# One-hot matmuls move the last chunk's rows into expert 0's slots; the kept slots are turned ahead of the ranks

## The reference

```
# 1. clustered attention: q, k, v (2, 8, 768, 64), 16 centroids per head
mask = argmax(q_n @ c_n) == argmax(k_n @ c_n)            # same nearest centroid
attn = softmax(where(mask, scale * q @ k.T, -1e9)) @ v    # -> x (1536, 512)
# 2. dense layer, w_in (512, 2048), w_out (2048, 512)
h = x @ w_in;  x = (h * sigmoid(1.702 * h)) @ w_out
# 3. mixture of 8 experts, two for each token, w1 (8, 512, 1024), w2 (8, 1024, 512)
noisy = x @ w_gate + log1p(exp(x @ w_noise)) * noise
top2 = two largest of noisy; weights = softmax of the two
out[token] = sum over its two experts of weight * (relu(x @ w1[e]) @ w2[e])
```

## Time and profile before

| | |
|---|---|
| median of 3 runs | 946.74 us (945.55 to 947.07) |
| the profiled execution's own time | 947.12 us |
| its span, first to last instruction | 945.3 us |
| mean granted TensorE clock | 0.971 of full |
| PE busy | 900.9 us, 95% of the span |
| DVE, ACT, POOL busy | 525.3, 420.4, 137.9 us |

### The profile page before, as it was taken

How to read it: one execution, slowest core, us unless ns; L and a number is a source line. 1 busy time by engine, 2 the same in 40 slices (tenths; PEclk the granted TensorE clock), 3 DMA queues, 4 the chain that set the end, 5 groups by cost and what they waited for, 6 DMA issues and landing times.

```text
span 945.3 us, 12455 instructions
## 1 busy us (share of the span) xinstructions
PE 900.9 (95%) x4314; PEld 732.3 (77%) x4315; DVE 525.3 (56%) x949; ACT 420.4 (44%) x685; POOL 137.9 (15%) x144
## 2 busy tenths in 40 slices
PE   6999999999999999999999991999999999999995
PEld 4777777777766888888888881888888888888884
DVE  7787878888755443456345533445344443444373
ACT  4667777676774332352235230424344243424320
POOL 2021221222121000005000504100000000005072
PEclk7999999999999999999999995899999999999998
DMA  5132432333174222325332534325263453428364
GB/s 121 38 92 75 124 92 52 120 90 94 41 236 165 97 89 89 134 90 178 90 133 89 179 109 150 130 90 175 85 206 114 146 178 116 166 89 285 121 220 146
DMA packets 84301, 118.98 MB, mean 126 GB/s; under 512 B 19258, under 2 KB 47930, under 8 KB 84256
## 3 DMA queue, kind: packets, MB, share of 16 engines
q1 hardware_dynamic: 79328, 104.08, 34.2%
q0 software_dynamic: 4928, 14.35, 4.4%
HBM read 89.12 MB, written 29.39 MB: 125 GB/s over the span
## 4 chain that ended last, share of the span: by engine, by line
PE 86%; DVE 8%; issue 2%; DMA 2%; ACT 1%; POOL 1%; SPq 0%; POOLq 0%; DVEq 0%; ACTq 0%
PE psum L867 10%; PE psum L868 10%; PE psum L869 10%; PE psum L881 9%; PE psum L783 9%; PE psum L882 9%; PE psum L883 9%; PE psum L748 3%; PE psum L768 3%; PE psum L769 3%; PE psum L1012 2%; DVE neg_max L1364 2%; PE psum L879 1%; PE psum L878 1%; PE psum L725 1%
## 5 line engine op out<-in xcount | busy, mean ns | idle before, releaser
L783 PE MATMUL psum<-probs,vx 128*128 128x386 f32 x384 | 155.8, 487 | 0.3 <-ACT probs L1078 0.3
L881 PE MATMUL psum<-down_hi,hid_hi 128*128 128x512 f32 x384 | 151.3, 394 | 0.0
L882 PE MATMUL psum<-down_lo,hid_hi 128*128 128x512 f32 x384 | 149.8, 390 | 0.0
L883 PE MATMUL psum<-down_hi,hid_lo 128*128 128x512 f32 x384 | 149.8, 390 | 0.0
L1243 ACT ACTIVATE hid_hi<-psum 128x448 fp32r<-128x448 f32 x64 | 34.8, 544 | 185.5 <-PE psum L869 185.5
L1078 ACT ACTIVATE probs<-psum 128x384 f32<-128x384 f32 x192 | 90.2, 488 | 54.9 <-PE psum L769 52.9
L1364 DVE TENSOR_REDUCE neg_max<-psum 128x1 f32<-128x768 f32 x96 | 91.3, 955 | 24.4 <-PE psum L748 20.7
L1646 DVE SCALAR_TENSOR_TENSOR hid_lo<-psum,hid_hi 128x384 fp32r<-128x384 f32 x64 | 35.6, 557 | 124.0 <-ACT hid_hi L1243 124.0
L1217 ACT ACTIVATE gelu<-psum 128x512 f32<-128x512 f32 x48 | 28.7, 598 | 158.9 <-PE psum L869 158.9
L867 PE MATMUL psum<-sx_hi,up_hi 128*128 128x448 f32 x256 | 94.7, 370 | 0.0
L868 PE MATMUL psum<-sx_lo,up_hi 128*128 128x448 f32 x256 | 94.5, 369 | 0.0
(11 more groups left out here) (194 smaller groups left out, 1495.1 us busy)
## 6 DMA issues: line engine op xcount, KB each, us to landing
raw<-in_moe_w SPq DMA_DIRECT2D x64, 512.0 KB, 4.3
raw<-in_moe_w_in SPq DMA_DIRECT2D x24, 512.0 KB, 3.4
raw<-in_moe_w_out SPq DMA_DIRECT2D x24, 512.0 KB, 5.1
slot_x<-zeros SPq DMA_DIRECT2D x7, 1024.0 KB, 5.5
slot_rows<-slot_x SPq DMA_DIRECT2D x8, 768.0 KB, 5.3
raw_q<-in_q SPq DMA_DIRECT2D x30, 192.0 KB, 3.4
raw_k<-in_k SPq DMA_DIRECT2D x30, 192.0 KB, 3.7
slot_y<-y_sb SPq DMA_DIRECT2D x7, 768.0 KB, 3.8
```

Of the source, the lines that this page charges most:

```text
L783: mm(psum[:, 5 + half, 0:WIDE], vx[:, n % 2, c], probs[:, at % SLOTS], start=(c == 0), stop=(c == J - 1)).then_inc(unit_done, 1)
L881: mm(dst, hid_hi[:, f % 2, cols], down_hi[:, slot, f % GP], start=(f == 0), stop=False)
L882: mm(dst, hid_hi[:, f % 2, cols], down_lo[:, slot, f % GP], start=False, stop=False)
L883: return mm(dst, hid_lo[:, f % 2, cols], down_hi[:, slot, f % GP], start=False, stop=(f == pieces - 1))
```

## The change

**Attention's end.** Of head 15's four splits, only the two of weight group 0 stand ahead of `head_result(15, 0)`; the two of group 1 come behind it.

**Expert 0's slots.** SP loads them after the last chunk's weight loads, when the low scatters of chunks 0 and 1 have landed (`slot_x` holds zeros in slots not yet taken). So `slot_rows` has the rows that the first two chunks put there. After the last chunk's `logits`, PE puts these "kept" slots in place with 16 matmuls against the identity (`kept_slots`, banks 4 to 7). They are ordinary float32 matmuls, no transposes, since the banks must go on accumulating. Then come the `ranks`. The last chunk's rows never go through DRAM for expert 0: ACT and DVE split `y_sb` into `row_hi` and `row_lo` (8 operations of 128x512, in the space of `xt_hi` and `xt_lo`); `first_moves` on DVE makes for each of the four tiles of tokens a matrix of ones and zeros (128 tokens by 448 slots) from `slot_of` and `key`; and `move_rows` on PE does 32 matmuls of 448 columns (4 blocks of features by 4 tiles by hi and lo) that add the rows to the banks. `place` comes behind `first_moves`; between its slot numbers and its weights DVE now does `turn_lo` for two of the four blocks, and for the other two at its end. The 16 transposes of expert 0's slots are gone.

**Queues.** POOL makes `slot_of` and waits for `sx_in` before it scatters the last chunk. SP's `expert_step` loads the next expert's slots behind the first two of its weight groups, not ahead of them, and first waits for all scatters.

**The end.** `hid_hi` and `hid_lo` get a third buffer for the last piece of the last expert; `down_end` takes the last three pieces tile by tile, and `ORDER` is 0, 3, 1, 2 everywhere.

```diff
--- before.py
+++ after.py
...
-        ORDER = (FULL,) + tuple(range(FULL))
+        ORDER = (0, FULL) + tuple(range(1, FULL))
...
+        def row_hi(j):
+
+            return xt_hi[:, j, 0:CT]
...
+        def moves(j):
+
+            return xt_hi[:, j, CT:CT + CAP]
...
-            keep_rows(t)
...
+            sp.wait_ge(scattered_low, (CHUNKS - 1) * (DMA * TPC))
+            load_slots(0, 0)
+            keep_rows(t)
+
             def expert_step(r, e, last):
                 n = r * E + e
                 if not last:
 
-                    when(sx_done, n * DC + DC)
-                    load_slots(r, e + 1)
                     for i in range(EGR):
+                        if i == STAGES:
+                            when(sx_done, n * DC + DC)
+                            sp.wait_ge(scattered_low, DMA * TILES)
+                            sp.wait_ge(scattered, DMA * TILES)
+                            load_slots(r, e + 1)
                         load_group(weights_of(e + 1, i), EXPERT0 + n * EGR + i + RING, i % STAGES)
...
-            sp.wait_ge(scattered_low, DMA * TILES)
-            load_slots(0, 0)
-            sp.wait_ge(scattered, DMA * TILES)
...
+
+            with pool.Fori(0, CHUNKS - 1) as t:
+                scatter_chunk(t)
+            chain.link(nc.gpsimd.iota(slot_i[:], pattern=[[1, CAP]], base=-FAR, channel_multiplier=0))
+            nc.gpsimd.tensor_copy(slot_of[:], slot_i[:]).then_inc(slot_of_set, 1)
+            pool.wait_ge(sx_in, 2 * DMA)
+            scatter_chunk(CHUNKS - 1)
...
-            def down_end(f, slot, piece, pieces):
...
+            def down_end(piece0, pieces):
+
                 for i, j in enumerate(ORDER):
-                    if i == 2:
-                        down_tile(f - 1, slot, True, ORDER[3], pieces)
-                    last = down_tile(f, slot, True, j, pieces)
-                    if i < TPC - 1:
+                    for f in range(pieces - 3, pieces):
+                        if i == 0:
+                            pe.wait_ge(hid_done, piece0 + f + 1)
+                        last = down_tile(f, f // GP % RING, True, j, pieces, 2 if f == pieces - 1 else None)
+                        if i == YT - 1 and f % GP == GP - 1:
+                            last.then_inc(group_used, 1)
+                    if i < YT - 1:
                         last.then_inc(y_ready, 1)
...
-                    if f >= 1:
+                    if f >= 1 and not (end and f == pieces - 2):
                         down(f - 1, ((f - 1) // GP) % RING, rest, piece0 + f - 1, pieces)
...
+                pe.wait_ge(sx_in, 2 * DMA)
+                for c in range(DC):
+                    kept_slots(c)
                 ranks(p, LAST)
+                for c in range(DC):
+                    move_rows(c)
+
+            def kept_slots(c):
+
+                for j in range(YT):
+                    rows = rows_of(j)
+                    mm(psum[:, turn_bank(c, True), j * P:j * P + rows], slot_rows[0:rows, j, c * P:(c + 1) * P],
+                       ident[0:rows, 0:rows], start=(j == 0), stop=False)
+
+            def move_rows(c):
+
+                dst = psum[:, turn_bank(c, True), 0:CAP]
+                for j in range(TPC):
+                    if c == 0:
+                        pe.wait_ge(split_lo, j + 1)
+                        pe.wait_ge(moves_ready, j + 1)
+                    mm(dst, row_hi(j)[:, c * P:(c + 1) * P], moves(j), start=False, stop=False)
+                    last = mm(dst, row_lo(j)[:, c * P:(c + 1) * P], moves(j), start=False, stop=(j == TPC - 1))
+                last.then_inc(sx_turned, 1)
...
-                turn_slots(r * E, 0, True)
-                turn_slots(r * E, 1, True)
+                if not end:
+                    turn_slots(r * E, 0, True)
+                    turn_slots(r * E, 1, True)
...
+                act.wait_ge(y_act, LEAD + 2 * p + 2)
+                act.wait_ge(y_dve, LEAD + 2 * p + 2)
+                for j in range(TPC):
+                    copy(row_hi(j), y_sb[:, j], ACT.Copy).then_inc(split_hi, 1)
                 softplus(p, LAST)
...
+                    held = 2 if end and f == FE // P - 1 else f % 2
...
+                    act.wait_ge(y_ready, (TPC - 1) * (CHUNKS + n) + ORDER.index(FULL) + 1)
...
-                    for x in range(4):
-                        split(0, x // 2, x % 2)
+                    for part in range(2):
+                        split(0, 0, part)
                 if n + 2 < HEADS:
                     row_max(n + 2, 0)
                 head_result(n, 0)
+                if n == HEADS - 1:
+                    for part in range(2):
+                        split(0, 1, part)
...
+                for j in range(TPC):
+                    dve.wait_ge(split_hi, j + 1)
+                    dv.tensor_tensor(row_lo(j), y_sb[:, j], row_hi(j).bitcast(F32), ALU.subtract)\
+                        .then_inc(split_lo, 1)
                 select(p, at, chain, LAST)
-                place(p, at, chain, LAST)
+                first_moves(p, chain, LAST)
+                def turn_half():
+
+                    for c in range(DC // 2):
+                        turn_lo(0, c, True)
+
+                place(p, at, chain, LAST, turn_half)
+                for c in range(DC // 2, DC):
+                    turn_lo(0, c, True)
+
+            def first_moves(p, chain, held):
+
+                chain.link(dv.scalar_tensor_tensor(out=key[:, 0], in0=r_one[:, 0, :, 0], scalar=-float(FAR),
+                                                   in1=base[:, 0:1].broadcast_to((P, TPC)), op0=ALU.mult, op1=ALU.add))
+                dve.wait_ge(slot_of_set, 1)
+                dve.wait_ge(rank_ready, p + 1)
+                chain.link(dv.tensor_tensor(
+                    key[:, 1], psum[:, held, RANK0:RANK0 + TPC * E].rearrange("p (j e) -> p j e", e=E)[:, :, 0],
+                    key[:, 0], ALU.add))
+                for j in range(TPC):
+                    dv.tensor_scalar(moves(j), slot_of[:], key[:, 1, j:j + 1], None, ALU.is_equal)\
+                        .then_inc(moves_ready, 1)
...
                 dve.sem_inc(slots_ready, 1)
+                if between:
+                    between()
...
+                    held = 2 if after and f == FE // P - 1 else f % 2
...
+                if not after:
+                    for c in range(DC):
+                        turn_lo(r * E, c, True)
...
```

More of the change, by code:

```diff
@@ L626, in _, with scatter_chunk @@
             pool.wait_ge(cleared, ALL_CLEARED)
-            with pool.Fori(0, CHUNKS) as t:
+            def scatter_chunk(t):
                 when(slots_ready, LEAD + t + 1)
@@ L870, in up, with down_tile @@
                 last.then_inc(hid_ready, 1)
-            def down_tile(f, slot, rest, j, pieces):
+            def down_tile(f, slot, rest, j, pieces, held=None):
+                held = f % 2 if held is None else held
                 dst = bank(j)
                 if rest and j == FULL:
-                    both = hid_hi[:, f % 2, j * P:]
+                    both = hid_hi[:, held, j * P:]
                     mm(dst, both, down_hi[:, slot, f % GP], start=(f == 0), stop=False)
@@ L880, in down_tile @@
                 cols = slice(j * P, (j + 1) * P)
-                mm(dst, hid_hi[:, f % 2, cols], down_hi[:, slot, f % GP], start=(f == 0), stop=False)
-                mm(dst, hid_hi[:, f % 2, cols], down_lo[:, slot, f % GP], start=False, stop=False)
-                return mm(dst, hid_lo[:, f % 2, cols], down_hi[:, slot, f % GP], start=False, stop=(f == pieces - 1))
+                mm(dst, hid_hi[:, held, cols], down_hi[:, slot, f % GP], start=(f == 0), stop=False)
+                mm(dst, hid_hi[:, held, cols], down_lo[:, slot, f % GP], start=False, stop=False)
+                return mm(dst, hid_lo[:, held, cols], down_hi[:, slot, f % GP], start=False, stop=(f == pieces - 1))
             def down(f, slot, rest, piece, pieces):
@@ L1493, in route, with turn_lo @@
                     place(p, at, chain, 6)
+            def turn_lo(n, c, first=False):
+                dve.wait_ge(sx_act, n * DC + c + 1)
+                dv.tensor_tensor(sx_lo[:, c], psum[:, turn_bank(c, first), 0:CAP], sx_hi[:, c].bitcast(F32), ALU.subtract)\
+                    .then_inc(sx_done, 1)
             def route_last(p, chain):
@@ L1534, in select, with place @@
                 dv.tensor_tensor(r_sel[:], r_one[:, 0], r_one[:, 1], ALU.add).then_inc(sel_ready, 1)
-            def place(p, at, chain, held):
+            def place(p, at, chain, held, between=None):
                 dve.wait_ge(rank_ready, p + 1)
@@ L1633, in _ @@
             PIECE0 = CHUNKS * (FF // P)
-            def turn_lo(n, c, first=False):
-                dve.wait_ge(sx_act, n * DC + c + 1)
-                dv.tensor_tensor(sx_lo[:, c], psum[:, turn_bank(c, first), 0:CAP], sx_hi[:, c].bitcast(F32), ALU.subtract)\
-                    .then_inc(sx_done, 1)
             def expert_step(n, last, kept, after=None):
@@ L1666, in experts @@
```

(5 more changed lines are left out.)

31 lines of the change are left out of this document (18 added, 13 removed).

## The result

The changed kernel takes 939.51 us (median of 4 runs, 937.07 to 940.87), beside 946.9 for the kernel before: a ratio of 0.9922 (95% interval 0.9899 to 0.9945). The gain is 7.4 us where 19.5 were forecast, and 939.5 is outside the range. The profiled execution took 940.87 us and its span is 939.1. Lines have moved: `up` is L899 to L901 now, `down` L914 to L916, the kept slots L1039, the moves L1049 and L1050.

The account below looks back on a forecast made before the run. TensorE, busy 95% of the span, was taken as the bound: gains only from its idling, removable work or lower clock. 3.75 + 13.85 + 1.9 = 19.5 us off 947.12 gave 927.6, stated as 927.5, range 924 to 933.

Parts of the forecast that it names:

- Part one: Attention's end: reordered splits remove PE's 2.05 us idle before the dense layer and 1.7 of half clock, together 3.75 us.
- attention's gain is given back: Rival, chance 0.06: the earlier first chunk waits for hidden halves of pieces 0 and 1; 931.3 us.
- Part two: Last chunk's route into expert 0: kept slots and moves replace the DRAM trip, piece 0 ends earlier; gain 13.85 us.
- the stall on `sx_lo` itself: Expert 0's first pieces: DVE's halves of blocks 2 and 3 come late for PE, 0.35 us of stall.
- the signs named for being wrong: Expert 0's route: a clock at 0.50 past 580, or `ranks` later than 577, would make the forecast wrong.
- 3.1 and 0.9: Kept slots at full clock: 3.1 us at twice a transpose per large matmul, plus 0.9 from the transposes' row; 3.9 stated.
- I let the kept slots count as wide: Clock in expert 0's route: kept slots count as wide matmuls from 569.4, so the clock rises at 573.7.
- the clock stays low through the moves: Rival, chance 0.20: half clock lasts through kept slots into the moves, piece 0 ends at 589.8; 931.4 us.
- four passes for float32: Kept slots by the skill's rule: 16 x 0.203 = 3.2 us plus 0.9, the sum 0.1 us worse.
- All this is hidden: POOL and SP queues: scatters some 3.5 us later, until about 592, and later slot loads cost nothing.
- Part three: The kernel's end: tile-by-tile finish starts the last scatter at 936.2 against 938.10, gain 1.9 us (1.1 to 2.9).

Follow-up runs that it names:

- e1: Only attention's reordered splits, against the kernel before: 945.26 us, ratio 0.9975.
- e4: The changed kernel run again unedited, in the first follow-up group: 940.33 us, ratio 0.9901 to the kernel before.
- e9: The changed kernel run again unedited, in the third follow-up group: 934.92 us, ratio 0.9868 to the kernel before.
- e13: The changed kernel run again unedited, in the fourth follow-up group: 934.04 us, ratio 0.9847 to the kernel before.
- e10: The changed kernel with the last chunk's scatters held until three pieces of expert 0 are done, second time: 929.70 us, ratio 0.9839 to the kernel before.
- e14: The changed kernel with the last chunk's scatters held until three pieces of expert 0 are done, third time: 934.74 us, ratio 0.9877 to the kernel before.
- e7: The changed kernel with the sixteen kept-slot matmuls issued as transposes: 929.75 us, ratio 0.9799 to the kernel before.
- e5: The changed kernel without the last chunk's eight scatters into `slot_x`: 932.99 us, ratio 0.9841 to the kernel before.
- e12: The changed kernel with kept slots as transposes and two unused matmuls after each tile's logits, eight in all: 932.41 us, ratio 0.9838 to the kernel before.
- e2: Only the new order at the end with the third buffer, against the kernel before: 945.81 us, ratio 0.9991.
- e8: The changed kernel with sixteen unused matmuls, two after each tile's logits and each c of the kept slots: 929.08 us, ratio 0.9806 to the kernel before.
- e6: The changed kernel with the last chunk's scatters held until three pieces of expert 0 are done, first time: 933.71 us, ratio 0.9844 to the kernel before.
- e17: The changed kernel with kept slots as transposes plus sixteen unused matmuls in logits and kept slots: 931.40 us, ratio 0.9839 to the kernel before.
- e3: The changed kernel with attention's and the end's edits taken back, leaving expert 0's route alone: 942.42 us, ratio 0.9951 to the kernel before.

## Why the prediction was wrong

The spans differ by 6.1 us; the forecast was 19.5. The 13.4 us between them, by the prediction's steps:

**Part one, 3.75: right in mechanism, 1.3 too large.** The first dense matmul came at 287.3 at full clock, as said. Over the sixteen profiles with this edit the first piece ends at 290.8 on average, over the four without it at 294.6: 3.8. Then 0.94 is given back before the turn (271.09 against 270.15), all of it between the ends of `up(1)` and `up(2)` of chunk 0. 0.67 of that is the wait for `hid_lo` of piece 0, whose subtraction was costed at 0.69 and took 1.39 beside GpSimd's last `pair_lo` (1.38 to 1.40 in all sixteen profiles with the edit, 0.69 in the four without); the other 0.27 I can't name. This is the rival "attention's gain is given back", with a sixth of its price. In this pair the changed kernel's last attention matmuls had also started 0.5 later to begin with (285.47 for 284.95). e1's 2.4 (1.3 to 3.4) agrees with 2.9.

**Part two, 13.85: the step that failed.** From the turn to the end of piece 0 the forecast has 22.0 us, the changed kernel took 26.2, in e4, e9 and e13 27.8. Cut at the steps: the kept slots were to take 6.0 (569.4 to 575.4) and took 8.76; `ranks` to the first move 1.3, took 1.48; the moves with their stall 6.85, took 7.9; the stall on `sx_lo` itself, 0.35, did not come. One of the signs named for being wrong did, a clock at 0.50 past 580. Two things are in it. The kept slots cost 4.9 us at full clock (e10) where I had 3.9 (3.1 and 0.9, so 4.0 by my own terms), and 8.8 at half where I had 7.5. And the sentence "I let the kept slots count as wide" was wrong: of the nine profiles that have the changed kernel's route, the clock fell in seven, in the logits or with the first kept slot; there it stayed at 0.50 through all the others and rose only 2.9 (changed) to 5.8 us (e13) into the moves. That is the rival "the clock stays low through the moves", to which I gave 0.20; its 931.4 us is still 2.6 to 3.5 below the changed kernel without late releases, as it had the kept slots too cheap as well. In e10 and e14 the clock did not fall, piece 0 ended after 20.7 us, and the spans were 926.7 and 927.8, where the forecast's is 925.8. So the forecast is near the kernel's time with a clock that it mostly does not have, and that by luck: it had 4.3 us of half clock in the route and these two have none.

On the price, the Trainium skill (FP8 and Floating Point Precision, TensorE Precision Notes) has four passes for float32, by which I had estimated 4.1. The trace has two records for each of these matmuls, not four, and 4.9 us in all: both estimates were low, that one by less. On the clock, the Trainium skill (TensorE: Matmul & The Clock Gate, Part 4) has it that transposes do not count as busy, from which I took that these matmuls would. The traces agree on transposes: in e7 the clock stayed at 0.50 over their 4.56 us. The matmuls did no better: they did not raise it in 8.8 us.

The text on the change says that the kept slots are no transposes "since the banks must go on accumulating". e7 shows that this was no reason: it transposes them into the open banks, and the moves add to what stands there.

**What was not in the forecast: 5.8 us behind piece 0.** From there to the end I had 1.9 less than before; it was 5.8 more. The 6.0 us of waits behind late releases and 3.4 us of half clock after the longest of them, worth 1.7, cover it. In the eleven profiles without late releases that have the new end, the same stages are 0.2 to 2.9 us shorter than in before, 1.7 on average. I costed GpSimd's later scatters at nothing ("All this is hidden"): right for the data that they move, but I did not ask what they run beside. What makes a release late stays open; that the scatters are its cause is not shown, only that it never came away from GpSimd's indirect DMAs.

**Part three, 1.9: right on average.** The sum of the last two columns is 345.48 in before and 343.5 to 343.9 in e9, e10, e13 and e14; over the eleven profiles just named it goes from 342.6 (e5) to 345.3 (e12). e2's 0.9 has an interval from a gain of 2.0 to a loss of 0.4.

So of the 13.4 us, 7.7 are behind piece 0, and are absent in the profiles of three of the six groups; 4.3 are part two (9.56 for 13.85), the kept slots and the clock; 1.3 are attention. Without late releases the changed kernel takes 934.0 to 934.9 us, 12.3 to 12.5 less than before beside it, still above the range.

**The better version.** e7 changes one argument of the changed kernel, which frees 4.3 us of TensorE at half clock, and has 0.9799. e8, which keeps the matmuls and holds the clock, has 0.9806. The changed kernel was not in their group; e6, which differs from it in the held scatters alone, is 4.0 and 4.6 us slower. Both together (e17) are 7.1 us faster than e7 in the one group where they ran side by side, most of it in late releases; in a group without late releases they were not tried.

## What to carry to other kernels

When a hole in the critical engine is filled with other work, price that work at the clock it will really have. Here the transposes, logits and kept slots did not keep the clock up in seven of nine profiles and brought it back in none, and sixteen unused matmuls (3.5 us) gave back more than they cost. Put float32 tiles in place by transposing them into the accumulation and not by multiplying with the identity, which took about twice as long (8.82 us against 4.56, both at half clock). And ask of every queue that the change sets beside a stage with little slack what it does when a release is late: repeat the kernel in several groups of runs before believing a difference of one per cent, because the kernel before may not feel what the changed one does.

## What the runs showed of the hardware

- A semaphore update of TensorE that ScalarE waits for came 0.3 to 7.9 us late 30 times in seven profiles (else ScalarE starts 0.04 us after the matmul), in three of six groups of runs, and only beside or up to 2.2 us behind GpSimd's indirect DMAs. The updates of the other engines in the same stretches of the changed kernel were not late. The DMA engines were not full meanwhile: busy for 0.38 of the time from 591 to 597. What sets it off I can't say.
- A 128x512 subtraction on VectorE took 1.39 us beside a 128x384 one of 1.20 us on GpSimd, against 0.69 alone.
- The sixteen float32 kept-slot matmuls take 0.31 us each at 2.4 GHz (e10) and 0.55 at 1.2, in two records; as transposes 0.28 at 1.2 (e7), in one, and later matmuls can add to what they left.
- The same route had the clock fall for 13.7 or 17.1 us in seven profiles (changed, e3 to e6, e9, e13), and not at all in two (e10, e14); e6, e10 and e14 are one kernel.
